# An RWKV block on one core: both batches in a stage, the first rows moved by TensorE, the first mix by batch

## What is computed

```
for t in range(S):
    cur = einsum('bhd,bhe->bhde', u * kt, vt)
    y[t] = einsum('bhd,bhde->bhe', rt, state + cur)
    state = wt * state + einsum('bhd,bhe->bhde', kt, vt)
x = y as (B, S, 384)
xk = mu_k * x + (1 - mu_k) * x_prev
xr = mu_r * x + (1 - mu_r) * x_prev
k = relu(xk @ w_k)
v = k * k @ w_v
x = sigmoid(xr @ w_r) * v
h = gelu(x @ w_in);  u, v = the two halves of h
v_n = (v - mean) / sqrt(var + 1e-6) * g_ln
gated = u * (w_sg @ v_n + b_sg)
out = x + gated @ w_out
```

## Time and profile before

| | before |
|---|---|
| median of 3 runs | 332.38 us (331.64 to 332.63) |
| the profiled execution | 332.15 us |
| its span | 330.4 us |
| mean granted clock of PE | 0.994 |
| PE busy | 320.4 us, 97% of the span |
| DVE / ACT / POOL busy | 60% / 46% / 30% |
| chain that ended last | PE 88%, DVE 4%, ACT 3%, DMA 2% |

### The profile page before, as it was taken

One profiled execution on the slowest core, in us unless ns is written; L12 is line 12 of the kernel. 1 busy time (PEld: TensorE's weight loads), 2 busy tenths in 40 slices (PEclk: granted clock), 3 DMA queues, 4 the chain that ended last, 5 costly groups with the idle time before them and its releaser, 6 DMA issues.

```text
span 330.4 us, 6795 instructions
## 1 busy us (share of the span) xinstructions
PE 320.4 (97%) x2682; PEld 300.5 (91%) x2682; DVE 197.7 (60%) x331; ACT 151.2 (46%) x301; POOL 97.7 (30%) x94
## 2 busy tenths in 40 slices
PE   6987999999999999999999999999999999999996
PEld 2656989999999999999999998899999989999996
DVE  4879999983696399639417065991643546123432
ACT  6448554544845455465547692755113025311100
POOL 5530343104314201430032050672333018313220
PEclk9999799999999999999999999999999999999999
DMA  7979043142304401300006046000000210000012
GB/s 234 407 260 370 4 137 130 70 138 60 137 3 163 167 4 28 140 9 2 8 10 237 0 131 233 22 0 0 2 0 0 97 49 2 0 0 2 0 48 95
DMA packets 11153, 28.09 MB, mean 85 GB/s; under 512 B 1232, under 2 KB 5872, under 8 KB 9840
## 3 DMA queue, kind: packets, MB, share of 16 engines
q1 hardware_dynamic: 10976, 27.51, 23.6%
q10 hardware_dynamic: 144, 0.14, 0.1%
HBM read 24.74 MB, written 2.36 MB: 82 GB/s over the span
## 4 chain that ended last, share of the span: by engine, by line
PE 88%; DVE 4%; ACT 3%; DMA 2%; issue 1%; POOL 0%; SPq 0%; ACTq 0%; DVEq 0%
PE dense L305 16%; PE dense L306 16%; PE dense L307 15%; PE ps L623 4%; PE pkt L650 3%; PE ps L306 3%; PE ps L307 3%; PE ps L305 3%; PE py L706 3%; PE py L692 2%; PE pu L673 2%; PE pkt L306 2%; PE pkt L305 2%; PE pkt L307 2%; PE pu L306 2%; PE pu L305 2%
## 5 line engine op out<-in xcount | busy, mean ns | idle before, releaser
L550 POOL TENSOR_TENSOR k_l<-sq,k_h 128x512 fp32r<-128x512 f32 x24 | 32.0, 1334 | 79.3 <-ACT sq L962 79.3
L305 PE MATMUL dense<-xkr_h,wk_h 128*128 128x256 f32 x144 | 42.4, 294 | 0.0
L305 PE MATMUL dense<-k_h,wv_h 128*128 128x256 f32 x144 | 41.3, 287 | 0.4 <-POOL k_l L550 0.4
L306 PE MATMUL dense<-xkr_l,wk_h 128*128 128x256 f32 x144 | 40.9, 284 | 0.0
L307 PE MATMUL dense<-xkr_h,wk_l 128*128 128x256 f32 x144 | 40.8, 284 | 0.0
L307 PE MATMUL dense<-k_h,wv_l 128*128 128x256 f32 x144 | 40.8, 283 | 0.0
L306 PE MATMUL dense<-k_l,wv_h 128*128 128x256 f32 x144 | 40.8, 283 | 0.0
L541 POOL TENSOR_TENSOR rkp<-inw 128x512 f32<-128x512 f32 x12 | 15.3, 1282 | 62.2 <-DVE r_in L1149 62.2
L954 ACT ACTIVATE relu<-dense 128x512 f32<-128x512 f32 x24 | 14.3, 596 | 35.8 <-PE dense L307 35.8
L603 POOL TENSOR_TENSOR gated_l<-gf,gated_h 128x384 fp32r<-128x384 f32 x16 | 16.4, 1023 | 46.5 <-ACT gated_h L1072 36.2
L305 PEld LDWEIGHTS dense<-xkr_h,wk_h 128*128 128x128 f32 x144 | 27.8, 193 | 1.0 <-issue 0.3
(11 more groups left out here) (247 smaller groups left out, 884.2 us busy)
## 6 DMA issues: line engine op xcount, KB each, us to landing
inw<-in_units SPq DMA_DIRECT2D x10, 1026.5 KB, 5.0
vb<-in_vT SPq DMA_DIRECT2D x12, 256.0 KB, 5.2
wsg_raw<-in_wsgT SPq DMA_DIRECT2D x1, 2304.0 KB, 8.5
out_y<-y_out SPq DMA_DIRECT2D x12, 192.0 KB, 1.9
wk_raw<-in_moe_w_k SPq DMA_DIRECT2D x3, 512.0 KB, 9.6
wv_raw<-in_moe_w_v SPq DMA_DIRECT2D x4, 384.0 KB, 7.3
win_raw<-in_moe_w_in SPq DMA_DIRECT2D x3, 512.0 KB, 4.7
inw<-in_units SPq DMA_DIRECT2D x2, 512.0 KB, 5.3
```

The costliest lines, as they stand in the source:

```text
L305: pe.matmul(o, a_h, b_h, start=first and n == 0, stop=False, skip_group_check=True)
L306: pe.matmul(o, a_h, b_l, start=False, stop=False, skip_group_check=True)
L550: pool.tensor_tensor(k2_l[:, 2 * n:2 * n + 2], sq[:, j % 2].rearrange("p (g t) -> p g t", g=2), k2_h[:, 2 * n:2 * n + 2], ALU.subtract).th ...
```

## The change

A stage is now one chunk of both batches: even units are batch 0, odd units batch 1, and `lay_out` puts the input in this order. `X` has a column of the step before for each batch. `from_state` is left out for units 0 and 1 (before: 0 and 6), `keys_by_step` and `add_state` for 10 and 11 (before: 5 and 11). Units 0 and 1 both have their fourth pair moved by PE, with no DMA. The r steps of the first mix are cut in two, by batch. The v tiles change places in every stage: `(2,)` comes first, and the waits for the squares' halves go with it. The hand-written orders of stages 0 and 1 are new on all engines; the first two `key_low` of stage 0 are DVE's (`EARLY` = 2), and POOL waits for `scores(2)` ahead of `products(2)` and for `scan(3)` ahead of its first `key_low`. SP loads `w_v` ahead of unit 3. Three of nine `warm` go. Batch 0's last 128 steps are split for the third part on their own (`XSPLIT`), as they are ready in stage 5 only. The orders of the stages 2 to 4 stay, but that `output` comes ahead of `carry_on`.

```diff
-        MOVED = 1
+        MOVED = range(N)
...
-            return un // N, *divmod(un, ST)
+            return un // N, un % N, un // N
...
-        VS = (("v", (0, 1)), ("v", (2,)))
+        VS = (("v", (2,)), ("v", (0, 1)))
...
+        R_MIXES = [(1, kt, slice(b, b + 1)) for kt in range(KT) for b in range(N)]
+        K_MIXES = [(0, kt, slice(0, N)) for kt in range(KT)]
+
+        def mixes(s):
+            return (R_MIXES if s == 0 else [(1, kt, slice(0, N)) for kt in range(KT)]) + K_MIXES
...
+        EARLY = 2
+
+        def key_lows(eng, j):
+
+            eng.wait_ge(k2le_done, min(j, EARLY))
+            if j > EARLY:
+                eng.wait_ge(k2l_done, j - EARLY)
...
+            pool.wait_ge(sc_mm, 3)
             products(2)
+            pool.wait_ge(rin_done, 4)
+            for n in range(EARLY, KG):
+                key_low(0, n)
             products(3)
...
-                    if kind == "v" and xs[0] == 0 and t % 2 == 0:
+                    if (kind, xs) == VS[0] and t % 2 == 0:
...
-            warm(pe, 2)
             scores(1)
-            bonus(0)
-            flag_of(0)
-            from_chunk(0)
-            bonus(1)
...
+            for un in range(N):
+                bonus(un)
+                from_chunk(un, last, last_mm)
+                from_chunk(un, main)
+            for un in MOVED:
+                move_last(un)
             keys_by_step(1)
-            pe.wait_ge(y_done, 1)
             pe.wait_ge(main_done, 1)
-            warm(pe, 2)
+            warm(pe, 1)
...
                     add_state(1)
-                    first_mlp(s, *KS[0])
+                    for tile in KS[:3]:
+                        first_mlp(s, *tile)
                     scores(a)
                     keys_by_step(a)
-                    first_mlp(s, *KS[1])
+                    first_mlp(s, *KS[3])
                     outputs(a)
                     scores(b)
                     keys_by_step(b)
+                    first_mlp(s, *VS[0])
                     flag_of(s + 1)
+                    outputs(b)
+                    first_mlp(s, *VS[1])
+                elif s == 1:
+                    for tile in RS + KS[:2]:
+                        first_mlp(s, *tile)
...
+            for un in range(N):
+                bonus(un)
+                last_output(un)
+            low_part(dve, parts_of("wk")[1], wl2_done)
+            for un in range(N):
+                main_output(un)
             dve.wait_ge(omu_done, 1)
+            dve.wait_ge(chosen, 1)
             mix(0)
-            scan(2)
             carry_on(1)
...
+                if s == 0:
+                    scan(a)
+                    low_part(dve, wv[0], wl2_done)
+                    key_low(0)
+                    mask(a)
...
+                    choose(s + 1)
+                    mix(s + 1)
+                    value(s, *VS[1])
+                    scan(a + 2)
...
-        b, c = divmod(un, S // C)
+        c, b = divmod(un, B)
```

More of the change, by code:

```diff
@@ L367, in filled2, with of_batch @@
             eng.wait_ge(n_full[n % NR], n // NR + 1)
+        XSPLIT = [(0, slice(0, S - C), range(STAGES - 1)), (0, slice(S - C, S), range(STAGES - 1, STAGES)),
+                  (1, slice(0, S), range(STAGES))]
+        def of_batch(b, at):
+            return slice(b * S + at.start, b * S + at.stop)
         def emptied2(eng, *tile):
@@ L757, in outputs @@
                 from_chunk(un)
+            main = range(PAIRS - 1)
+            last = range(PAIRS - 1, PAIRS)
             warm(pe, 4)
@@ new lines, in mix @@
+            def mix(s):
+                todo = mixes(s)
+                if s:
+                    dve.wait_ge(chosen, s + 1)
+                    given(dve, s)
+                    if s >= 2:
+                        dve.wait_ge(xf_done, mix_count(s - 2, *todo[-1]))
+                    dve.tensor_copy(X[:, s % 2, :, :, 0:1], X[:, (s - 1) % 2, :, :, C:C + 1]).then_inc(prev_done, 1)
+                dve.wait_ge(prev_done, s + 1)
+                mix_now(s, *todo[0])
+                for i in range(1, len(todo)):
+                    mix_now(s, *todo[i])
+                    mix_low(s, *todo[i - 1])
+                    if s == 0 and i == len(R_MIXES):
+                        carry_on(0)
+                        low_part(dve, parts_of("wk")[2], wl2_done)
+                mix_low(s, *todo[-1])
@@ L1269, in _ @@
                     bonus(a)
-                    carry_on(a)
                     output(a)
                     mask(b)
-                    if s == 0:
-                        low_part(dve, wv[1], wl2_done)
+                    carry_on(a)
+                    value(s, *VS[0])
+                    bonus(b)
+                    output(b)
+                    carry_on(b)
+                    choose(s + 1)
+                    mix(s + 1)
+                    value(s, *VS[1])
+                    scan(a + 2)
+                elif s == 1:
+                    scan(b)
+                    mask(a)
+                    bonus(a)
+                    output(a)
+                    carry_on(a)
+                    mask(b)
+                    scan(a + 2)
+                    value(s, *VS[0])
+                    bonus(b)
+                    output(b)
+                    carry_on(b)
+                    mask(a + 2)
+                    choose(s + 1)
+                    mix(s + 1)
+                    scan(b + 2)
+                    value(s, *VS[1])
+                elif s < STAGES - 1:
+                    bonus(a)
+                    output(a)
+                    carry_on(a)
+                    mask(b)
@@ L1288, in _ @@
                         scan(b + 2)
+                    for tile in VS:
+                        value(s, *tile)
                 else:
@@ L1291, in _ @@
                         low_part(dve, j, wl2_done)
-                    for kt in range(KT):
-                        split_x2(0, kt)
-                for tile in VS:
-                    value(s, *tile)
+                    split_x2(0)
+                    for tile in VS:
+                        value(s, *tile)
+                    split_x2(1)
             def normalise(n):
@@ L1315, in _ @@
                 if kind == "x":
-                    for kt in range(KT):
-                        split_x2(b, kt)
+                    split_x2(2)
                 elif kind == "v":
```

340 lines of the change are left out of this document (181 added, 159 removed).

## The result

The changed kernel takes 344.0 us (median of 6 runs, 342.62 to 344.78), the kernel before 332.15 us in the runs beside it (6, 331.64 to 332.63). The ratio is 1.035, 95% interval 1.033 to 1.0375: slower, by 11.9 us, where 9.2 were forecast. The profiled execution is the fastest of the six, 342.62 us with a span of 340.9. It is the one in which PE's granted clock never fell. The other five have a mean clock of 0.99 or 0.995 over the span and lie 1.2 to 2.2 us above it. So of the 11.9 us some 10.5 are waits and order, which the profile shows, and the other 1.4 goes with the clock, which it does not show.

The account below looks back on a forecast made before the run. PE was taken as the bound, working 320.4 of the span's 330.4 us. The terms summed to +6.95 us, with the clock +9.2, so 332.15 + 9.2 = 341.3 us, range 337.0 to 345.0.

Parts of the forecast that it names:

- 1 opening, to the first k tile: Stage 0's opening: DVE blocked behind POOL, mix earlier but halved steps eat the gain; first k tile ends at 30.5, -0.3 us.
- 2 wait for the scores of unit 2: Stage 0: three k tiles ahead of these scores remove PE's 2.1 us wait and 1.75 of slow clock, -3.85 us.
- 3 waits of unit 3 in stage 0: Stage 0: PE waits for DVE at unit 3's scores, +1.5 us, and its transposes wait for unit 2's bonus, +0.4.
- 4 border to stage 1: Between stages 0 and 1: one v tile just covers the DMAs, but the first k tile waits for its bank, +0.9 us.
- 5 one more from_state: PE's own work inside the stages: one from_state more, +0.9 us.
- 6 short v tile first, stages 1 to 4: Start of the v tiles: PE wants POOL's last low half too early, 1.33 us lost per stage, +5.3 us.
- 6 the same, stage 5: Stage 5's v tiles: PE stops for 0.8 and 1.9 us, with more matmuls left afterwards, +2.1 us.
- 7 clock: PE's clock falls behind idle gaps: 1.75 us in stage 5, 0.5 in the opening; +2.2 us, between 0 and 4.5.
- the rival of a shared port: Opening: DVE and POOL share the port, so the low half ends 1.2 us earlier; 339.6 us, chance 0.08.
- part 1's own rule: Opening: the port pair shared by GpSimd and VectorE is an exclusive lock; DVE is blocked until POOL is done at 19.81.
- a further wait in the new orders: Rival, stages 0 and 1: a slip where ACT reaches unit 2's keys adds to all; 346 us or more, chance 0.05.
- Part 7's own worst case: Clock falls at their largest: 1.05 us in the opening, 1.75 in stage 5, 1.75 at unit 3's wait in stage 0.

Follow-up runs that it names:

- e1: Kernel before with only the v tiles changed, the short one ahead of the long one in all six stages: 340.22 us, ratio 1.024.
- e12: Changed kernel, long v tile first in stages 2 to 5, POOL's stage 1 wait, DVE's scan of unit 3, bonus and state of unit 2 earlier: 335.94 us.
- e4: Changed kernel with POOL waiting for DVE's scan of unit 5 ahead of its first low half of stage 1: 342.16 us, ratio 1.029.
- e3: Kernel before with the second k tile of stage 0 ahead of the scores of unit 2, the others moved up: 329.89 us, ratio 0.993.
- e2: Changed kernel with the long v tile first again in stages 2 to 5: 337.07 us, ratio 1.016.
- e5: Changed kernel with the r steps of the first mix whole again, not halved by batch: 344.5 us, ratio 1.038.

## Why the prediction came out as it did

The sign, the place and the size of the largest term were right, and 344.0 lies in the range. The sum was 2.7 us short. Without the clock it was 3.5 short, 6.95 against 10.5, and a term for the clock that was 0.8 too large hid a part of that. By its parts:

| part | forecast | profile of after |
|---|---|---|
| 1 opening, to the first k tile | -0.3 | +0.1 (28.54 against 28.47) |
| 2 wait for the scores of unit 2 | -3.85 | gone: -2.1, and 1.6 of slow clock |
| 3 waits of unit 3 in stage 0 | +1.9 | +2.0 (1.67 + 0.35) |
| 4 border to stage 1 | +0.9 | +1.1 (0.57 + 0.52) |
| 5 one more from_state | +0.9 | +1.0 |
| 6 short v tile first, stages 1 to 4 | +5.3 | +5.8 (1.53 + 3 x 1.15 in the list, and 4 x 0.2) |
| 6 the same, stage 5 | +2.1 | +2.1 |
| missed: mask in stage 1 | 0 | +1.0 |
| missed: stage 2, 0.23 and 0.32 | 0 | +0.55 |
| 7 clock | +2.2 | 0 here, +1.4 in the median |

- **Part 6 was right, and shown by itself** (e1). It was read from when POOL's row ends against when the tile wants it. Only stage 1 was off, 1.53 for 1.15 in the others: `k_l` took 1.64 us beside DVE's `r_in`.
- **What I priced too low is the stop itself.** The list counts idle time from the modelled end of the last matmul, 0.28 us after its start; the next one would have started 0.12 after it. So a wait of 1.15 in the list cost 1.37 in e1's table, 0.2 more than its row. Part 6 had been worked out from starts and holds that. The last column adds up to +10.0 of the 10.5 seen; what the smaller waits cost beyond their rows is of the size of the 0.5 left, and was not measured by itself.
- **Part 1 booked a gain that its own steps do not give.** The full block (DVE's low half `17.85 2.97`, ended 20.82, forecast 20.95) and the first matmul (23.66, forecast 23.75) were right; the rival of a shared port is out. The third block came at 25.95 with a stop of 0.31, forecast 25.85. But by the prediction's own count the r tiles end at 27.65 against 27.6 before, so nothing was gained there, and no row stands behind the 30.5 and 30.8 from which the 0.3 was taken. Measured, what follows the r tiles starts at 27.92 (before 27.86), the first k tile at 28.54 (28.47).
- **Part 4: the DMAs were taken at their old time.** I took 2.8 us from the last output to ACT's start, the value before. It was 3.5 from the issue alone in after, and 5.0 in e12. Part of this was a wait of 0.57 that the sum does not have; why it was 3.5 and not 2.8 with the load over stays open. The bank wait was 0.52, forecast 0.9.
- **The missed wait** is that of part 1's own rule in another place: I used it in the opening, and did not look for POOL's new neighbours on DVE in stage 1, where the change moved a scan beside them. e4 shows it: stage 1 is 1.6 us shorter without it, 1.0 of that is the wait at the mask and 0.3 the shorter one for `k_l`. Among the rivals, a further wait in the new orders had 0.05, at ACT in stage 0 and with 346 or more; it came true in kind, in another place and at another price.
- **Parts 2 and 7, the clock.** The fall behind the wait of 2.09 us was real (from the scores of unit 2 to those of unit 3 it is 8.81 us before and, without its wait, 7.2 in e1) but free, as it covered the late mask. In after the mask is in time and the 1.6 came in; in e1 and e3 it did not. Part 7's two places were right, as e2 and e5 (opening) and e4 (stage 5) show, but not that they fall in every execution, and the wait of part 3, taken at 0, was a third (1.4 us in e4). Where the clock fell in the five slower executions of after is not known, as only their mean is.
- **That 344.0 lies in the range owes something to luck.** Part 7's own worst case, 4.55 for 2.25, adds 2.3 to 341.3 and gives 343.6; the prediction added 3.7 without saying for what. The upper bound had no room for waits that were forgotten, and these made the 344.0.

## What to carry to other kernels

Ask of a tile order not only how much work it is but after how many instructions it wants its last input: one row of the producer's timeline against the consumer's start gave two thirds of this loss before anything ran. Take the good part of a large change alone: a second tile ahead of one wait gave 0.7%, and all the rest of it cost 4%. And where a feeding engine has no gap, a wait that is reordered away comes back at its next product; follow it until a gap takes it in.
